# Attention inside a fused attention and two-layer MLP kernel: the product with v in fp32, 64 columns for each head, in place of three fp32r passes over 128 columns

## The chip, the cores and the metric

The kernel is written in Bass for one core of a Trainium2 chip. The core has TensorE (PE: matmuls and transposes), VectorE (DVE), ScalarE (ACT), GpSimd (POOL) and the queues of SyncE (SP), which issues the DMAs. The metric is the device time of one execution in microseconds (us). Two times are compared as medians over several runs.

## The reference

What is computed, for B = 4 batches, H = 8 heads, S = 576 positions, D = 64, all float32:

```python
scores = scale * np.matmul(q, k.transpose(0, 1, 3, 2))        # per batch and head, 576 x 576
x = (log1p(|i - j|) / log1p(max(i, 1)))[..., None]
bias = np.maximum(x @ w1 + b1, 0.0) @ w2                       # (576, 576, 8), the same for every batch
scores = scores + bias.transpose(2, 0, 1)[None]
attn = softmax(scores, axis=-1)                                # with 1e-9 added to the sum
x = np.matmul(attn, v)                                         # then (B*S, H*D) = (2304, 512)
h = np.maximum(np.maximum(x @ moe_w1, x @ moe_w2), x @ moe_w3) # 2304 x 768
y = h @ moe_w_out                                              # 2304 x 512
out = gelu_like(y @ moe2_w_in) @ moe2_w_out                    # inner width 2048, piecewise quadratic
```

## The kernel before, in words

The kernel has four stages that follow one another: the bias for all heads (to about 63 us), attention (to about 423 us), the first MLP and the second MLP. The change touches attention alone.

TensorE knows two ways of multiplying 32-bit numbers here. An fp32r operand is a number rounded to fewer bits; a product of two of them is one matmul. To keep precision, a number x is split into `hi` (x rounded) and `lo` (x minus hi, rounded), and a product is the sum of `hi*hi`, `hi*lo` and `lo*hi`. An fp32 operand goes in whole, and the trace shows two matmul records for one such product.

**Pairs and steps.** A (batch, head) is called a pair here, m = 0 to 31, and two neighbours (m even and odd) have the same batch and adjoining heads; i = m // 2 counts these. All engines run `step(m, par, i)` for m = -1 to 34, with par = m % 2. Steps -1 to 3 and 30 to 34 are written out, and steps 4 to 29 are a loop over i with two steps in its body (`steps`); in the loop semaphores are waited on against register values, and `carry` adds one `sem_inc` on several engines.

**One step on TensorE** is five tiles of query rows, t = 0 to 4 (the last has 64 rows). For each t, in order:

- scores of pair m: four matmuls of 288 columns (L1043), k_hi and k_lo against `q_s`, where `q_s` holds hi of q in partitions 0 to 63 and lo of q in 64 to 127. They all write the one place `score_ps()`, so each tile waits until DVE has read the tile before (`s_bias`);
- transposes of the normalised probabilities of pair m-1, four of 128x128 into one PSUM bank (L1055, slot `p0` to `p4`);
- at t = 0, 1, 2, transposes of q and k of pair m+1 (L975, L1071, slots `q`, `k`, `qk`), whose inputs `q_dup` and `k_dup` hold each row twice side by side;
- a share of the product with v (`output_share`, `outputs`, L988). `v_hi` and `v_lo` hold, for a block kt of keys, v of both heads with a zero block between them, so that a stationary 128x128 operand has v of one head in its own 64 columns and zeros in the other's. Nine such blocks (four for each head, and one in which the tails of both heads lie in 64 partitions each) times three passes times two column halves (256 and 320 columns, PSUM banks 6 and 7) make 54 matmuls for two pairs. They are dealt over t = 2, 3, 4 of the even step m = 2i and over t = 0 to 4 of the odd step that follows. After an even step come four transposes of the collected tails (`tail`, L1079).

The transposes use four PSUM banks, 2 to 5, by the tables `T_BANKS`; `before` finds the slot that held a bank last, and `open_slot` waits until DVE is done with it.

**The other engines.** DVE adds bias to the scores and finds the minimum (L818, two buffers `s_sb`, so it also waits for the exp two tiles ago). ACT takes the exp (L635). POOL normalises the probabilities (L512) and copies their last 64 columns to `p_tail` (L518). Each transposed slot is rounded by ACT to hi (`high`, L616) and then DVE subtracts to get lo (`low`, L802, for lo of q L804). POOL writes `q_dup` and `k_dup` (`dup`, L503) and splits v to `v_hi` (L530) and `v_lo` (L533). ACT copies finished outputs to `xT` (L653, L657). SP loads q and k two pairs ahead, v one double pair at a time into one buffer, and at each change of heads the bias (`load_bias`, L356).

Of the kernel before, what the change touches and what calls it, by code (L numbers as in the profile page):

```python
# [20 lines left out]
F32 = mybir.dt.float32  # L21
# [3 lines left out]
ds = bass.ds  # L25
# [5 lines left out]
def build(nc, q, k, v, w1, b1, w2, moe_w1, moe_w2, moe_w3, moe_w_out, moe2_w_in, moe2_w_out, out):  # L31
# [41 lines left out]
    with ctx:  # L73
# [9 lines left out]
        with att:  # L83
# [18 lines left out]
            v_hi = sb("v_hi", [P, 3 * T + 2, D], F32R, c=att)  # L102
            v_lo = sb("v_lo", [P, 3 * T + 2, D], F32R, c=att)
# [8 lines left out]
            p_hi = sb("p_hi", [P, 2, T, S], F32R, c=att)  # L112
            p_lo = sb("p_lo", [P, 2, T, S], F32R, c=att)
            pt_hi = sb("pt_hi", [P, S], F32R, c=att)
            pt_lo = sb("pt_lo", [P, S], F32R, c=att)
# [4 lines left out]
        with moe:  # L120
# [16 lines left out]
        O_AT = (3, 1)  # L137
# [21 lines left out]
        vv_in = sem("vv_in")  # L159
        dup_ok = sem("dup_ok")  # L160
        v_hi_ok = sem("v_hi_ok")
        v_ok = sem("v_ok")
        t_ps = sem("t_ps")
        t_hi = sem("t_hi")
        t_lo = sem("t_lo")
        tail_ps, tail_hi, tail_lo = sem("tail_ps"), sem("tail_hi"), sem("tail_lo")
# [35 lines left out]
        ORDER = ("p0", "q", "p1", "k", "p2", "qk", "p3", "p4")  # L202
        T_BANKS = (dict(zip(ORDER + ("tail",), (2, 3, 4, 5, 2, 3, 4, 5, 2))),
                   dict(zip(ORDER, (3, 4, 5, 2, 4, 5, 3, 4))))
        QK_ONLY = ("q", "k", "qk")
        P_ONLY = tuple(n for n in ORDER if n not in QK_ONLY)
        Q_AT, K_AT, QK_AT = 0, 1, 2

        def order_of(m):

            if not isinstance(m, int):
                return ORDER
            return QK_ONLY if m < 1 else P_ONLY if m >= PAIRS - 1 else ORDER

        def filled(m):

            if isinstance(m, int):
                return sum(len(order_of(n)) for n in range(-1, m))
            return len(ORDER) * m + (filled(4) - len(ORDER) * 4)

        def slot(m, name):

            return filled(m) + order_of(m).index(name)

        def before(m, par, i, name):


            bank = T_BANKS[par][name]
            names = order_of(m) + (("tail",) if par == 0 and later(m, 2) else ())
            earlier = names[:names.index(name)]  # L230
            while True:
                for n in reversed(earlier):
                    if T_BANKS[par][n] == bank:
                        return (tail_lo, i) if n == "tail" else (t_lo, slot(m, n) + 1)
                m, i, par = m - 1, i if par else i - 1, 1 - par
                if isinstance(m, int) and m < -1:
                    return None
                earlier = order_of(m) + (("tail",) if par == 0 and later(m, 2) else ())

        def steps(eng, body):  # L240

            def peeled(m):
                body(m, m % 2, m // 2)

            for m in range(-1, 4):
                peeled(m)
            with eng.Fori(2, PAIRS // 2 - 1) as i:
                body(2 * i, 0, i)
                body(2 * i + 1, 1, i)
            for m in range(PAIRS - 2, PAIRS + 3):  # L250
                peeled(m)

        def has(m, lag):

            return not isinstance(m, int) or 0 <= m - lag < PAIRS

        def later(m, first):

            return not isinstance(m, int) or m >= first
# [43 lines left out]
        passed = {name: sem(f"{name}_passed") for name in ("pe", "dve", "pool", "sp")}  # L303

        def carry(eng, m, name):


            if not isinstance(m, int):
                eng.sem_inc(passed[name], 1)

# [3 lines left out]
        def _(sp):  # L314
# [18 lines left out]
            def load_qk(b, hp, e, first=False):  # L333

                m = 2 * (B * hp + b) + e
                if not first:
                    sp.wait_ge(dup_ok, m - 1)
                    carry(sp, m, "sp")
                load(q, q_in, b, 2 * hp + e, e, qk_in[e], "(p t) d -> p t d")
                load(k, k_in, b, 2 * hp + e, e, qk_in[e], "(t p) d -> p t d")  # L340

            def load_v(b, hp):

                if not (isinstance(b, int) and b == 0 and hp == 0):
                    sp.wait_ge(v_ok, B * hp + b)
                    if not isinstance(b, int):
                        carry(sp, b, "sp")
                for h in range(2):
                    sp.dma_start(v_in[:, 2 * h:3 * T:3, :],
                                 v[b, 2 * hp + h, 0:MAIN, :].rearrange("(t p) d -> p t d", t=T)).then_inc(vv_in, 16)  # L350
                    sp.dma_start(v_in[h * HALF:(h + 1) * HALF, 3 * T + h, :],
                                 v[b, 2 * hp + h, MAIN:S, :]).then_inc(vv_in, 16)

            def load_bias(hp, e):
# [3 lines left out]
                sp.dma_start(bias_h[0:HALF, e, T, :], bias_d[MAIN:S, h, :]).then_inc(bias_in[e], 16)  # L358

            load_qk(0, 0, 0, True)  # L360
            load_qk(0, 0, 1, True)
            load_v(0, 0)


# [826 lines left out]
```

## Time and profile before

| | |
|---|---|
| median of 3 runs | 1139.0 us (1138.79 to 1141.09) |
| profiled execution, its own time | 1139.37 us |
| its span in the profile | 1137.6 us |
| granted TensorE clock, mean | 0.99 of full speed |
| steps 2 to 31 | one double step, even and odd, in 21.3 us |

The span is the time from the first to the last instruction on the core. A record of a matmul has a modelled end, which lies after the start of the next; so the time that a matmul takes in a stream is read from the distance between two starts, and from the share that says "busy" nothing can be read on how well TensorE is used.

### The profile page before, as it was taken

How to read it: one execution, taken by the hardware profiler on the slowest of the kernel's cores; microseconds unless marked ns; L12 is line 12 of the kernel's file. 1: busy time of each engine (PE TensorE's matmuls, PEld its weight loads, DVE VectorE, ACT ScalarE, POOL GpSimd, SP SyncE). 2: the span in 40 equal slices, each digit the busy share in tenths (PEclk: the TensorE clock that was granted, in tenths of full speed). 3: DMA queues.
4: the chain of work that ended last, by engine and by line, in shares of the span. 5: the costliest groups of instructions: out<-in, count | busy, mean ns of one | idle time of the engine just before them, and what ended most of it. 6: DMA issues, size and time to landing. Idle time of an engine off the chain costs nothing.

```text
span 1137.6 us, 21240 instructions
## 1 busy us (share of the span) xinstructions
PE 1091.7 (96%) x6872; PEld 998.1 (88%) x6872; DVE 632.1 (56%) x1441; ACT 575.0 (51%) x1210; POOL 341.9 (30%) x544
## 2 busy tenths in 40 slices
PE   6869999999999979999999999999999999999997
PEld 2358899899899879999999999999899989989996
DVE  8958888888888852323222222475444444444543
ACT  7957887887887853312121122464334343433432
POOL 5027767767767737400000003481000000000000
PEclk9979999999999999999999999999999999999999
DMA  4551141141141114200000002140101000010101
GB/s 136 210 186 42 48 130 42 47 130 42 47 130 42 28 32 131 93 1 1 0 0 0 0 0 75 56 130 1 29 1 28 0 17 11 0 28 0 29 1 28
DMA packets 80774, 55.30 MB, mean 49 GB/s; under 512 B 44896, under 2 KB 66400, under 8 KB 80736
## 3 DMA queue, kind: packets, MB, share of 16 engines
q1 hardware_dynamic: 80736, 54.82, 16.4%
q8 instruction: 21, 0.34, 0.1%
q14 instruction: 17, 0.14, 0.0%
HBM read 39.46 MB, written 15.34 MB: 48 GB/s over the span
## 4 chain that ended last, share of the span: by engine, by line
PE 86%; issue 2%; DVE 2%; POOL 1%; ACT 1%; ACTq 0%; DVEq 0%
PE ps L1095 37%; PE ps L1139 18%; PE ps L988 11%; PE ps L1043 7%; PE ps L1107 7%; PE ps L1055 5%; DVE s_sb L818 1%; PE ps L975 1%; PE ps L1071 1%; PE ps L1079 1%; ACT probs L635 0%; POOL w_lo L563 0%; DVE row_min L818 0%; POOL v_lo L533 0%; POOL probs L512 0%
## 5 line engine op out<-in xcount | busy, mean ns | idle before, releaser
L1095 PE MATMUL ps<-x_hi,w_hi 128*128 128x384 f32 x816 | 274.4, 336 | 3.8 <-DVE x_lo L860 3.5
L1095 PE MATMUL ps<-x_hi,w_lo 128*128 128x384 f32 x816 | 274.3, 336 | 0.0
L1095 PE MATMUL ps<-x_lo,w_hi 128*128 128x384 f32 x816 | 273.8, 336 | 0.0
L563 POOL TENSOR_TENSOR w_lo<-raw,w_hi 128x256 fp32r<-128x256 f32 x108 | 83.6, 804 | 274.4 <-ACT w_hi L671 274.2
L1095 PEld LDWEIGHTS ps<-x_hi,w_hi 128*128 128x128 f32 x816 | 153.8, 188 | 8.6 <-issue 3.7
L1095 PEld LDWEIGHTS ps<-x_lo,w_hi 128*128 128x128 f32 x816 | 153.6, 188 | 3.9
L1095 PEld LDWEIGHTS ps<-x_hi,w_lo 128*128 128x128 f32 x816 | 153.5, 188 | 0.0
L818 DVE CUSTOM_DVE_ANT_0 s_sb<-ps,bias_h 128x576 f32<-128x576 f32 (+1 forms) x160 | 120.3, 752 | 43.8 <-PE ps L1043 24.5
L512 POOL TENSOR_SCALAR probs<-probs,row_inv 128x512 f32<-128x512 f32 (+1 forms) x160 | 108.3, 692 | 91.6 <-DVE row_inv L792 91.6
L635 ACT ACTIVATE probs<-s_sb,row_min 128x576 f32<-128x576 f32 (+1 forms) x160 | 124.3, 777 | 19.2 <-DVE row_min L818 18.3
L616 ACT ACTIVATE p_hi<-ps 128x512 fp32r<-128x512 f32 (+1 forms) x160 | 88.7, 555 | 58.4 <-PE ps L1055 46.0
L1139 PE MATMUL ps<-w_hi,g_lo 128*128 128x512 f32 x288 | 113.9, 395 | 0.0
L1139 PE MATMUL ps<-w_lo,g_hi 128*128 128x512 f32 x288 | 113.6, 395 | 0.0
L1139 PE MATMUL ps<-w_hi,g_hi 128*128 128x512 f32 x288 | 112.6, 391 | 0.0
L802 DVE TENSOR_TENSOR p_lo<-ps,p_hi 128x512 fp32r<-128x512 f32 (+1 forms) x160 | 101.0, 632 | 8.1 <-ACT p_hi L616 5.6
L727 ACT ACTIVATE ta<-ps 128x384 f32<-128x384 f32 x96 | 47.0, 490 | 115.7 <-PE ps L1095 115.0
L907 DVE TENSOR_SCALAR tb<-ta 128x384 f32<-128x384 f32 x96 | 38.0, 396 | 113.9 <-ACT ta L727 112.1
L874 DVE TENSOR_TENSOR tb<-ps,ta 128x384 f32<-128x384 f32 x36 | 20.1, 557 | 144.5 <-PE ps L1095 144.5
L1055 PE MATMUL ps<-ident,probs 128*128 128x128 f32 (+1 forms) x640 | 92.5, 267 | 1.1 <-DVE p_lo L802 1.1
L1043 PE MATMUL ps<-k_hi,q_s 128*128 128x288 f32 (+1 forms) x320 | 75.8, 319 | 15.6 <-DVE row_min L818 13.3
L915 DVE TENSOR_TENSOR g_lo<-tb,g_hi 128x384 fp32r<-128x384 f32 x96 | 56.9, 593 | 58.5 <-ACT g_hi L737 58.5
L988 PE MATMUL ps<-p_hi,v_hi 128*128 128x256 f32 (+1 forms) x256 | 86.1, 336 | 1.4 <-POOL v_lo L533 1.4
(104 smaller groups left out, 2029.3 us busy)
## 6 DMA issues: line engine op xcount, KB each, us to landing
bias_scratch<-probs SPq DMA_DIRECT2D x36, 288.0 KB, 2.1
bias_h<-bias_scratch SPq DMA_DIRECT2D x7, 1152.0 KB, 5.9
raw<-in_moe_w_out SPq DMA_DIRECT2D x22, 256.0 KB, 3.0
raw<-in_moe_w SPq DMA_DIRECT2D x18, 256.0 KB, 3.0
out<-o_sb SPq DMA_DIRECT2D x36, 128.0 KB, 2.4
q_in<-in_q SPq DMA_DIRECT2D x32, 128.0 KB, 2.0
k_in<-in_k SPq DMA_DIRECT2D x32, 128.0 KB, 2.4
v_in<-in_v SPq DMA_DIRECT2D x32, 128.0 KB, 2.3
```

Source lines behind the costliest of these rows:

```text
L512: pool.tensor_scalar(pr, pr, row_inv[0:rows[t], par, t:t + 1], 1.0, ALU.mult, ALU.mult).then_inc(p_norm, 1)
L563: last = pool.tensor_tensor(w_lo[:, at + c:at + c + PIECE], raw[:, u % 2, c:c + PIECE], w_hi[:, at + c:at + c + PIECE].bitcast(F32), ALU.s ...
L616: last = act.activation(dst, src, ACT.Copy, scale=scale)
L635: act.activation(probs[0:n, par, t, :], s_sb[0:n, (par + t) % 2, :], ACT.Exp, scale=-1.0, bias=row_min[0:n, par, t:t + 1], accum_out=row_s ...
L802: last = dve.tensor_tensor(dst, src, hi.bitcast(F32), ALU.subtract)
L818: dve.tensor_tensor_reduce(halves(s_sb[0:n, (par + t) % 2, :]), score_ps()[0:n], halves(bias_h[0:n, par, t, :]), 1.0, 3.0e38, ALU.add, ALU ...
L988: last = pe.matmul(ps[:, bank, 0:cols.stop - cols.start], vx[:, at:at + 2, :].rearrange("p a d -> p (a d)"), tx[:, cols] if h is None else ...
L1043: last = pe.matmul(score_ps()[0:n, c, :], q_s[:, par, t * P:t * P + n], kx[:, par, c * HC:(c + 1) * HC], start=(part == 0), stop=(part == 1))
L1055: last = pe.transpose(ps[:, bank, c * n:(c + 1) * n], pr[:, c * P:(c + 1) * P], ident[0:n, 0:n])
L1095: last = pe.matmul(ps[:, bank, 0:BLK], w[:, at:at + P], x[:, kt, :], start=(kt == 0 and n == 0), stop=(kt == KT - 1 and n == 2))
L1107: last = pe.matmul(ps[:, Y_BANK + dt, 0:BLK], w[:, at:at + P], g[:, ft % 2, :], start=(opens and i == 0), stop=(closes and i == 2))
L1139: last = pe.matmul(ps[:, O_BANK + t, :], g[:, ft % 4, t * P:(t + 1) * P], w[:, wout_d(ft):wout_d(ft) + DM], start=(opens and i == 0), stop ...
```

## The change: what it does

- **The product with v** takes `v_in` as it is loaded and the transposed probabilities, both in fp32. Head 0 has a stationary operand of 128x64 that writes PSUM partitions 0 to 63, head 1 another that writes 64 to 127, in turn. Five blocks of keys (the last is the tail, with zeros in v for the other head's partitions) times two heads times two column halves make 20 products, 40 records, for two pairs. They are dealt by `SHARES`: t = 2 has block 0, t = 3 blocks 1 and 2, t = 4 blocks 3 and 4; the 256-column half in the odd step 2i+3, the 320-column half in the even step 2i+4, one step later than before.
- **p is copied, not split.** `p0` and `p2` are copied by ACT alone, `p1`, `p3`, `p4` and `tail` by DVE alone, to `p_t` and `pt_t`, which have two buffers. The v split on POOL is gone.
- **q is split ahead of its transpose.** POOL writes hi of q (320 elements a partition) to one half of `q_dup`, duplicates k as before, and subtracts to get lo of q in the other half. After the transpose ACT alone writes `q_s`; DVE's subtraction for q is gone. k is split as before.
- **Steps are written out**, all 36 of them, with constants in every wait. The four banks go round in the order of the slots; a slot waits for the copy of the slot four before it, on a count of ACT's or DVE's (`t_act`, `t_dve`).
- **SP** loads v into two buffers and waits for the outputs of the double pair before the last (`o_ps`); this wait stands ahead of the loads of q and k and of the bias in its queue.

The core of the diff:

```diff
-            v_in = sb("v_in", [P, 3 * T + 2, D], c=att)
+            v_in = sb("v_in", [P, 2, 2, NT, D], c=att)
-            p_hi = sb("p_hi", [P, 2, T, S], F32R, c=att)
-            p_lo = sb("p_lo", [P, 2, T, S], F32R, c=att)
+            p_t = sb("p_t", [P, 2, 2, T, S], c=att)
+            pt_t = sb("pt_t", [P, 2, S], c=att)
+        SHARES = {2: (0,), 3: (1, 2), 4: (3, 4)}
...
+        BY_ACT = ("p0", "p2", "q", "k", "qk")
+        BY_DVE = ("p1", "p3", "p4", "tail", "k", "qk")
+        SLOTS = [(m, name) for m in STEPS for name in names_of(m)]
+        T_BANKS = 4
+        def t_bank(m, name):
+            return 2 + SLOT[m, name] % T_BANKS
...
+            def load_v(i):
+                if i >= 2:
+                    sp.wait_ge(o_ps, 2 * (i - 2) + 2)
...
+            for i in range(PAIRS // 2):
+                if i:
+                    load_v(i)
+                for e in range(2):
+                    if i + 2 < PAIRS // 2:
+                        load_qk(2 * (i + 2) + e)
+                    if i % B == B - 1 and i + 1 < PAIRS // 2:
+                        sp.wait_ge(s_bias, NT * (2 * i + e + 1))
+                        load_bias((i + 1) // B, e)
...
+                pool.tensor_scalar(q_dup[:, par, :, 0, :].bitcast(F32R), q_in[:, par, :, :], 1.0, 1.0,
+                                   ALU.mult, ALU.mult).then_inc(q_hi_ok, 1)
+                pool.tensor_scalar(k_dup[:, par, :, :, :],
+                                   k_in[:, par, :, :].unsqueeze(2).broadcast_to([P, NT, 2, D]), 1.0, 1.0,
+                                   ALU.mult, ALU.mult)
+                pool.wait_ge(q_hi_ok, m + 1)
+                pool.tensor_tensor(q_dup[:, par, :, 1, :], q_in[:, par, :, :], q_dup[:, par, :, 0, :],
+                                   ALU.subtract).then_inc(dup_ok, 1)
...
-                    pool.tensor_scalar(v_hi[:, :, :], v_in[:, :, :], 1.0, 1.0, ALU.mult, ALU.mult).then_inc(v_hi_ok, 1)
-                    pool.tensor_tensor(v_lo[:, :, :], v_in[:, :, :], v_hi[:, :, :].bitcast(F32),
-                                       ALU.subtract).then_inc(v_ok, 1)
...
-                        if t == Q_AT + 1:
-                            qs = q_s[HALF:P, e, 0:MAIN]
-                            low("q", [(qs, ps[HALF:P, T_BANKS[par]["q"], 0:MAIN], -SCALE, qs)])
...
+                    if has(m, 1) and f"p{t}" in BY_DVE:
+                        src = ps[:, t_bank(m, f"p{t}"), :]
+                        i = (m - 1) // 2
+                        last = copy(f"p{t}", p_t[:, i % 2, e, :, t * P:t * P + n],
+                                    src[:, 0:T * n].rearrange("p (c n) -> p c n", c=T))
...
+                def outputs(i, half, kts):
+                    bank, cols = O_BANKS[half]
+                    for kt in kts:
+                        if kt == 0:
+                            if half == 0:
+                                pe.wait_ge(vv_in[i % 2], 64 * (i // 2 + 1))
+                                pe.wait_ge(t_act, ACT_COUNT[2 * i + 2, "p2"])
+                                pe.wait_ge(t_dve, DVE_COUNT[2 * i + 2, "tail"])
+                            if i >= 1:
+                                pe.wait_ge(o_ok, 2 * (i - 1) + half + 1)
+                        for h in range(2):
+                            last = pe.matmul(ps[h * HALF:(h + 1) * HALF, bank, 0:cols.stop - cols.start],
+                                             v_in[:, i % 2, h, kt, :],
+                                             pt_t[:, i % 2, cols] if kt == T else p_t[:, i % 2, h, kt, cols],
+                                             start=(kt == 0), stop=(kt == T))
+                    if kts[-1] == T:
+                        last.then_inc(o_ps, 1)
...
+                    if par == 1 and has(m, 3):
+                        outputs((m - 3) // 2, 0, SHARES[t])
+                    if par == 0 and has(m, 4):
+                        outputs((m - 4) // 2, 1, SHARES[t])
...
+            for m in STEPS:
+                step(m)
```

## Rows read from the trace of the kernel before

**Rows 1.** The page: busy engines, and the granted clock in 40 slices.
```profile
PE 1091.7 (96%) x6872; PEld 998.1 (88%) x6872; DVE 632.1 (56%) x1441; ACT 575.0 (51%) x1210; POOL 341.9 (30%) x544
PEclk9979999999999999999999999999999999999999
```

**Rows 2.** Windows: stretch, busy us of each engine (instructions), granted clock, DMA.
```profile
200.00:300.00 100.00, 98.22 (x752) 91.21 (x752) 87.01 (x225) 81.10 (x199) 72.00 (x123) 1.00 0.25 69
88.00:92.00 4.00, 2.90 (x21) 2.35 (x22) 3.22 (x11) 2.73 (x7) 3.69 (x7) 1.00 0.01 4
```

**Rows 3.** Timeline of PE, scores at four tiles: start, us, operation, count.
```profile
200.09 0.53 PE L1043 MATMUL ps<-k_hi,q_s 128*128 128x288 f32 x2 [0.20 <-DVE row_min L818]
...
217.68 0.49 PE L1043 MATMUL ps<-k_hi,q_s 128*128 128x288 f32 x2
...
219.53 0.54 PE L1043 MATMUL ps<-k_hi,q_s 128*128 128x288 f32 x2 [0.22 <-DVE row_min L818]
...
221.40 0.53 PE L1043 MATMUL ps<-k_hi,q_s 128*128 128x288 f32 x2 [0.20 <-DVE row_min L818]
```

**Rows 4.** Timeline of DVE: the tile of scores of 219.53 as DVE takes it.
```profile
220.59 0.75 DVE L818 CUSTOM_DVE_ANT_0 s_sb<-ps,bias_h 128x576 f32<-128x576 f32 x1
```

**Rows 5.** Timeline of PE, tiles 1, 2 and 3 of an odd step.
```profile
209.87 0.60 PE L1055 MATMUL ps<-ident,probs 128*128 128x128 f32 x4
210.30 0.60 PE L975 MATMUL ps<-ident,k_dup 128*128 128x128 f32 x4
...
211.62 0.42 PE L1043 MATMUL ps<-k_hi,q_s 128*128 128x288 f32 x2
...
212.15 0.60 PE L1055 MATMUL ps<-ident,probs 128*128 128x128 f32 x4
212.68 0.27 PE L1071 MATMUL ps<-ident,q_dup 64*128 64x64 f32 x1
212.79 0.22 PE L1071 MATMUL ps<-ident,k_dup 64*128 64x64 f32 x1
212.95 0.39 PE L988 MATMUL ps<-pt_hi,v_hi 128*128 128x256 f32 x1
213.17 0.28 PE L988 MATMUL ps<-pt_lo,v_hi 128*128 128x256 f32 x1
213.29 0.29 PE L988 MATMUL ps<-pt_hi,v_lo 128*128 128x256 f32 x1
...
214.38 0.60 PE L1055 MATMUL ps<-ident,probs 128*128 128x128 f32 x4
...
215.11 0.31 PE L988 MATMUL ps<-p_hi,v_lo 128*128 128x320 f32 x1
215.25 0.31 PE L988 MATMUL ps<-p_hi,v_hi 128*128 128x320 f32 x1
```

**Rows 6.** Timeline of PE, one tile of the bias stage, into four column groups.
```profile
58.03 1.30 PE L948 MATMUL ps<-xT,w2b 128*32 128x288 f32 x16 [0.29 <-ACT xT L583]
```

**Rows 7.** Groups by line, 200 to 300 us, of DVE and POOL.
```profile
L802 DVE TENSOR_TENSOR p_lo<-ps,p_hi 128x512 fp32r<-128x512 f32 x38 | 26.1, 686 | 0.3
L804 DVE SCALAR_TENSOR_TENSOR q_s<-ps,q_s 64x512 fp32r<-64x512 f32 x10 | 7.0, 695 | 0.3
L533 POOL TENSOR_TENSOR v_lo<-v_in,v_hi 128x896 fp32r<-128x896 f32 x5 | 10.6, 2110 | 0.9 <-POOL v_hi L530 0.9
L503 POOL TENSOR_SCALAR q_dup<-q_in 128x640 f32<-128x640 f32 x10 | 7.2, 720 | 0.0
```

**Rows 8.** Timeline of PE at the end of attention.
```profile
412.37 0.51 PE L988 MATMUL ps<-p_hi,v_hi 128*128 128x256 f32 x1 [1.35 <-POOL v_lo L533]
...
422.67 0.31 PE L988 MATMUL ps<-pt_hi,v_lo 128*128 128x320 f32 x1
426.48 0.66 PE L1095 MATMUL ps<-x_hi,w_hi 128*128 128x384 f32 x1 [3.50 <-DVE x_lo L860]
```

**Rows 9.** Timeline of the SP queue at a change of heads.
```profile
227.77 0.57 SPq L356 DMA_DIRECT2D bias_h<-bias_scratch  x1
```

More of the change, by code:

```diff
@@ L215, in filled @@
[L215 to L251, printed above, removed]
-        def has(m, lag):
-            return not isinstance(m, int) or 0 <= m - lag < PAIRS
-        def later(m, first):
-            return not isinstance(m, int) or m >= first
+        STEPS = range(-1, PAIRS + 3)
@@ new lines, in build, with names_of @@
+        Q_AT, K_AT, QK_AT = 0, 1, 2
+        BY_ACT = ("p0", "p2", "q", "k", "qk")
+        BY_DVE = ("p1", "p3", "p4", "tail", "k", "qk")
+        def has(m, lag):
+            return 0 <= m - lag < PAIRS
+        def names_of(m):
+            for t in range(NT):
+                if has(m, 1):
+                    yield f"p{t}"
+                if has(m, -1) and t in (Q_AT, K_AT, QK_AT):
+                    yield {Q_AT: "q", K_AT: "k", QK_AT: "qk"}[t]
+            if m % 2 == 0 and has(m, 2):
+                yield "tail"
@@ L607, in _, with step, turned, output @@
                 bias_copy(s, s % 4, NSUP // 4 - 1)
-            def step(m, par, i):
+            def step(m):
+                par = m % 2
                 e = 1 - par
-                def high(name, outs):
-                    act.wait_ge(t_ps, slot(m, name) + 1)
-                    for dst, src, scale in outs:
-                        last = act.activation(dst, src, ACT.Copy, scale=scale)
-                    last.then_inc(t_hi, 1)
+                def turned(name):
+                    act.wait_ge(t_ps, SLOT[m, name] + 1)
+                    return ps[:, t_bank(m, name), :]
+                def output(i, half):
+                    bank, cols = O_BANKS[half]
+                    act.wait_ge(o_ps, 2 * i + half + 1)
+                    act.activation(xT_flat[:, i * S + cols.start:i * S + cols.stop],
+                                   ps[:, bank, 0:cols.stop - cols.start], ACT.Copy).then_inc(o_ok, 1)
@@ L663, in _ @@
-            steps(act, step)
+                            src = turned("qk")
+                            act.activation(q_s[:, e, MAIN:S], src[:, 0:HALF], ACT.Copy, scale=-SCALE)
+                            act.activation(k_hi[:, e, MAIN:S], src[:, HALF:2 * HALF], ACT.Copy).then_inc(t_act, 1)
+                    if t == O_AT:
+                        if par == 0 and has(m, 4):
+                            output(m // 2 - 2, 0)
+                        if par == 1 and has(m, 5):
+                            output((m - 1) // 2 - 2, 1)
@@ L664, in _ @@
+            for m in STEPS:
+                step(m)
+            output_last = PAIRS // 2 - 1
+            bank, cols = O_BANKS[1]
+            act.wait_ge(o_ps, PAIRS)
+            act.activation(xT_flat[:, output_last * S + cols.start:output_last * S + cols.stop],
+                           ps[:, bank, 0:cols.stop - cols.start], ACT.Copy).then_inc(o_ok, 1)
             act.wait_ge(o_ok, PAIRS)
@@ L854, in _ @@
-            steps(dve, step)
+                            last = dve.tensor_copy(pt_t[:, i % 2, MAIN:S], src[:, T * n:NT * n])
+                        last.then_inc(t_dve, 1)
+            for m in STEPS:
+                step(m)
             dve.wait_ge(o_ok, PAIRS)
@@ L1080, in step @@
                                             p_tail[:, t, :, :].rearrange("p a d -> p (a d)"), ident[:, :])
-                    last.then_inc(tail_ps, 1)
-            steps(pe, step)
+                    last.then_inc(t_ps, 1)
+            for m in STEPS:
+                step(m)
             pe.wait_ge(o_ok, PAIRS)
```

278 lines of the change are left out of this document (83 added, 195 removed).

## The prediction

> **What bounds the kernel now.** I read the page first. TensorE is busy for 96% of the span and no other engine for more than 56% [rows 1]. In the attention stage, which is all that the change touches, the windows show a PE that is 98% busy, with DVE at 87%, ACT at 81% and POOL at 72%, at full clock [rows 2]. So the stage hangs on TensorE, but three engines are close behind. Whether a busy PE is working or waiting is read from the starts in its timeline. Scores at the same tile of two even steps start at 200.09 and 221.40 us: a double step takes 21.31 us [rows 3]. The stage has 15 of them in steady state (steps 2 to 31), 320 us of the 1137.6.
>
> Two kinds of tile make up a double step. At tiles 0 and 1 of an even step PE has no product with v to do, and it waits for DVE: the starts are 1.85 and 1.87 us apart, with an idle time put down to row_min each time [rows 3]. This is a loop: scores (0.53 us of PE when nothing hinders them, 211.62 to 212.15 [rows 5]), then DVE starts on them, then PE may write the next. DVE took the scores of 219.53 at 220.59 and PE went on at 221.40 [rows 3, 4], so from DVE's start to PE's next start 0.81 us pass. At the other eight tiles the products with v fill the time and PE goes from one thing to the next.
>
> **The change part by part.**
>
> *The products removed.* Starts of neighbouring passes are 0.12 us apart for 256 columns (213.17 to 213.29) and 0.14 to 0.15, I take 0.145, for 320 columns (215.11 to 215.25) [rows 5]. 27 of each for a double step: 3.24 + 3.92 = 7.2 us.
>
> *The products added.* In fp32 a record streams at half the rate: four transposes of 128 columns take 209.87 to 210.30, 0.43 us, so 0.107 us for 128 columns of one record [rows 5]. A product is two records, so 256 columns take 0.43 us and 320 take 0.53. Alone, 20 products would be 10 x (0.43 + 0.53) = 9.6 us, more than what goes. Side by side on their own columns the two heads would be half, 4.8 us. The nearest row for that is the bias stage: eight fp32 products of 288 columns, 16 records into four groups of 32 columns, stand in 1.30 us [rows 6]. At the rate just found one record of 288 is 0.24 us and 16 in a row 3.84 us. So column groups do run beside one another, with different moving data, in the same bank. That was four groups of 32; two of 64 is the same thing at another width, and I take 4.8 us.
>
> *What a change of tiling costs.* This is the unknown. The trace shows a change of row tiling: transposes of 128 rows from 212.15 end their stream at 212.58, and those of 64 rows start at 212.68, 0.10 later. They end at about 212.85; the third pass of the product behind them starts at 213.29, 0.44 later, where two passes are 0.24: 0.20 to get back to 128x128. Where no tiling changes, transposes from 214.38 end at 214.81 and the third pass starts at 215.11, 0.30 for two of 0.145, so nothing [rows 5]. So I price a share of the product with v, entered and left, at 0.10 + 0.20 = 0.30 us. There are six shares in a double step (tiles 2, 3 and 4, twice). At tiles 2 and 4 a change out of 64 rows is there already and merges with the new one. The bounds: 0 if 64-column tiles need no change, and 0.55 if, besides, the second head trails the first by a record (0.21 to 0.27) at the end of each share.
>
> The Trainium skill, "TensorEngine Tiling (Array Packing)", Key Properties, speaks against the change here: another tile of the same mode is free, but a new mode drains TensorE. It has no figure for that; the 0.10 and 0.20 above agree with it, for rows. By its table of theoretical speedup (up to 2x for a dimension of 64) alone, the products would take 4.8 us and the changes nothing.
>
> *The new double step.* The rows give transposes 0.43, the pair of small transposes with the step into 64 rows 0.27 (212.58 to 212.85), scores 0.53, or 0.63 after a wait for DVE, when the weights are not in ahead (an estimate: 1.87 between the two waiting starts of rows 3 is 0.63 of scores, 0.43 to the start on DVE, and 0.81). The last tile, with its 64-row transposes, is 0.95 without products, by my reading of the same timeline, and 0.43 more for the tails in the even step.
> - Tiles 0 and 1 in both steps are now in the loop with DVE. Before, the tile at 219.53 lost about 0.1 because DVE was still at the last lo. That work is gone, so 1.80 in place of 1.86: 4 x 1.80 = 7.20.
> - Even step, 320 columns: tile 2 has 0.63 + 0.43 + 0.27 + 0.53 + 0.30 = 2.16; tile 3 has 0.96 + 1.07 + 0.30 = 2.33; tile 4 has 0.95 + 0.43 + 1.07 + 0.30 = 2.75. Together 7.24.
> - Odd step, 256 columns: 2.06, 2.11 and 2.10, together 6.27.
>
> In all 20.7 us. In the same way of counting the old step comes out 0.1 low (a wait here and there), so I take 20.85, which is 0.46 less than 21.31. Times 15: -6.9 us. The 2.4 us that the streams save per double step are given back as 1.8 of tiling changes, and as tiles 0 and 1 of the odd step, whose products used to cover the loop with DVE and now don't.
>
> *DVE* loses two of five p_lo (0.69 each) and the lo of q (0.70 and a small one) each step [rows 7]; the rest become copies, for which I take the subtraction's time. From 87% of 10.66 us, 9.3, it goes to about 7.1 in a step of 10.4. *ACT* loses p1, p3, p4 and the tail and has less to do as well. *POOL* loses v_lo (2.11 every second step) and v_hi [rows 7]. For q it gains a rounding of 320 elements and a subtraction of 320, which by v_lo's rate is 0.75, and loses the 0.72 of q_dup: about +0.5 a step against -1.5. All of this is behind TensorE and costs or gives nothing, beyond the 0.06 in the loop. What waits on POOL (p_norm for tile 0 of the next step) had over a microsecond to spare.
>
> *The written-out steps* drop register arithmetic and one sem_inc an engine. The steps written out already are not visibly quicker except for about 0.1 at tile 0; I take 0. A bigger program means more fetching of instructions; nothing in the trace bounds that, 0 again.
>
> *SP.* The wait on o_ps now stands before eight DMA issues, some 0.55 us each by the row of another (0.57), and at a change of heads before the bias. Bias went out at 227.77 for a step that began at 239.0 and its data took some 6 us [rows 9]. It will go out about 4.5 us later, with a step that is shorter by 0.2: some 1 us is left. Three such places; cost 0, at worst 3 x 1 us.
>
> *The ends.* At the start the second tile waits for the bias, whatever else; 0 to -0.7, I take -0.3. At the end PE waited for v_lo before 412.37, ran the passes until 422.67 plus 0.15, partly at half clock, and the MLP began at 426.48 [rows 8]. Now nothing waits for v, and after the last transposes there are 4.8 us of products, of which the first half waits for the copy of the tails (about 1.3 us). I take -2.5, between 0 and -4.
>
> Sum, against the profiled execution's 1139.4: -6.9 - 0.3 - 2.5 = -9.7, so 1129.7. It stands 0.4 above the median; that makes 1129.
>
> **The rivals.**
> 1. *Changing the tiling costs nothing.* Then a double step has tiles of 1.80 (the loop holds all but two), 2.03 and 2.5: about 19.0 us. 15 x -2.3 - 3 gives 1102. For it: the scores of the last tile, labelled 128*64, come behind 128*128 products with no gap. Against: those are fp32r at position 0, and may not be tiled at all; and the row tiles do pay. Cases in between, at 0.15 a share, give 1115.
> 2. *The second head trails and the drain is dearer*, 0.6 us a share. Six times 0.3 more than I took: 22.6 us, 15 x 1.3 - 3 gives 1156. It decides from about 0.40 a share, where the time is as before. For it: the bias tile's last record starts 0.89 after its first (1.30 less 0.41 for the record itself), where four rounds of 0.24 would have 0.72 [rows 6]; so the groups do not start together.
> 3. *The two heads do not overlap at all* (the other side, and far). 4.8 us more per double step: 25.6, 15 x 4.3 - 2 gives about 1200. Against it stands rows 6 alone. The Trainium skill, "TensorE: Matmul & The Clock Gate", What overlaps and what doesn't, says that weight loads overlap matmuls only when the row group differs; here both heads have the same rows. Taken at its word, with loads of 64 columns exposed, this would be rival 2 or 3; rows 6 has one row group as well, and overlaps.
> 4. *The clock.* PE has more gaps, and the granted clock could fall to 1.2 GHz, as in the drain. At 88 to 92 us PE is busy for 2.9 us of 4 and the clock stays at 1.00 [rows 2]. If it fell for good, well over 1200.
>
> **How the numbers follow.** Forecast, 0.2 to 0.45 us a share: 0.50. Rival 1: 0.24. Rival 2: 0.14. Rival 3: 0.10. Rival 4: 0.02. The forecast's own range is 1121 to 1139. For the range over all, rival 3 and 4 and the far end of rival 1 stay outside: 1103 to 1152. Within 0.2% (2.3 us), about what a measurement of this kernel can tell from no change, are the top of the forecast's band and the bottom of rival 2: 0.12. Faster: rival 1 and most of the band, 0.68. Slower: 0.20.
>
> **What would show it.** In the profile after: two records of 256 columns for each head with starts that make 0.43 us a block, not 0.85; gaps of 0.1 before and 0.2 after each share; scores at tiles 0 and 1 of both steps 1.8 us apart with an idle time before them that ends on row_min; even steps longer than odd ones, by about 1 us; no wait of DVE for bias. The prediction is wrong if a share costs much more or less than 0.3, or if PE waits for a bank, for p_norm or for v.

## The result, and the profile after

The changed kernel takes 1124.1 us (median of 4 runs, 1122.6 to 1125.5) against 1139.3 us of the kernel before beside it: a ratio of 0.9864, 95% interval 0.9851 to 0.9876. It is 15.2 us faster, where 10 were forecast; 1124.1 lies inside the whole range and inside the forecast's own 1121 to 1139.

The page of the changed kernel, whose profiled execution took 1122.62 us with a span of 1120.8:

```profile
PE 1076.4 (96%) x6648; PEld 918.9 (82%) x6648; DVE 559.7 (50%) x1313; ACT 515.2 (46%) x1082; POOL 312.7 (28%) x544
PEclk9979999999999999999999999999999999999999
```

By its share PE is as busy as in [rows 1], and the clock is the same. Only windows over the attention stage tell the two apart (stretch, busy us of PE, PEld, DVE, ACT, POOL, granted clock, DMA share and GB/s):

```profile
200.00:300.00 100.00, 98.35 (x710) 70.93 (x708) 68.22 (x196) 66.07 (x168) 66.10 (x128) 1.00 0.27 72
```

Beside [rows 2], DVE went from 87 to 68, ACT from 81 to 66, POOL from 72 to 66. PE is "98% busy" in both and says nothing; its weight loads fell from 91 to 71. What the stage takes is read from the starts. PE in the changed kernel, an odd step from 200.40, then an even one from 210.05 (start, us, operation, count):

```profile
200.40 0.51 PE L955 MATMUL ps<-k_hi,q_s 128*128 128x288 f32 x2
...
202.13 0.53 PE L955 MATMUL ps<-k_hi,q_s 128*128 128x288 f32 x2
...
203.78 0.53 PE L955 MATMUL ps<-k_hi,q_s 128*128 128x288 f32 x2
...
205.79 0.53 PE L955 MATMUL ps<-k_hi,q_s 128*128 128x288 f32 x2
...
206.43 0.60 PE L967 MATMUL ps<-ident,probs 128*128 128x128 f32 x4
206.96 1.08 PE L927 MATMUL ps<-p_t,v_in 128*64 128x256 f32 x8
207.97 0.48 PE L955 MATMUL ps<-k_hi,q_s 128*64 128x288 f32 x2
...
208.65 0.46 PE L967 MATMUL ps<-ident,probs 64*128 64x64 f32 x4
...
210.05 0.53 PE L955 MATMUL ps<-k_hi,q_s 128*128 128x288 f32 x2
...
211.80 0.53 PE L955 MATMUL ps<-k_hi,q_s 128*128 128x288 f32 x2
...
213.45 0.53 PE L955 MATMUL ps<-k_hi,q_s 128*128 128x288 f32 x2
...
215.57 0.54 PE L955 MATMUL ps<-k_hi,q_s 128*128 128x288 f32 x2
...
217.97 0.48 PE L955 MATMUL ps<-k_hi,q_s 128*64 128x288 f32 x2
...
220.73 0.51 PE L955 MATMUL ps<-k_hi,q_s 128*128 128x288 f32 x2
```

The double step takes 20.33 us (200.40 to 220.73), 0.98 less than the 21.31 of [rows 3]. Its ten tiles, against the prediction's terms:

| tile | odd: forecast, measured | even: forecast, measured |
|---|---|---|
| 0 | 1.80, 1.73 | 1.80, 1.75 |
| 1 | 1.80, 1.65 | 1.80, 1.65 |
| 2 | 2.06, 2.01 | 2.16, 2.12 |
| 3 | 2.11, 2.18 | 2.33, 2.40 |
| 4 | 2.10, 2.08 | 2.75, 2.76 |

A share of the product can be read at 206.96. The transposes before it end their stream at 206.43 + 0.43 = 206.86, so the way in costs 0.10. Two blocks of 256 columns are 0.85 us, scores 0.53 and the step into 64 rows 0.09; from 206.96 to 208.65 are 1.69, which leaves 0.22 for the way out. At tile 2 (205.21, not shown) the same sum leaves 0.27. A share costs 0.32 to 0.37, where I took 0.30. What the time of the way out is spent on is not shown: about 0.10 of it lies between the first two pairs of scores behind a share, and scores that have waited for DVE, with no change of tiling before them, show the same 0.10.

Where the 16.8 us between the two spans (1137.6 and 1120.8) come from, by starts of PE in both traces:

| stretch | before | after | difference |
|---|---|---|---|
| first scores to the start of step 3 | 34.0 | 31.2 | -2.8 |
| steps 3 to 30, 14 double steps | 298.2 | 286.8 | -11.4 |
| step 31 to the first matmul of the MLP | 27.8 | 25.2 | -2.5 |
| the rest | 777.6 | 777.6 | 0.0 |

The first row is in part chance. Its steps 0 and 1 take 22.8 us here, but 24.1 in the profile of bias_first and 21.9 in that of tail_moved (both below), whose code for these steps is nearly the same; in this stretch the granted clock changes between its two levels at different places (at 75 to 79 us it is 0.87 before and 0.50 after, at 82 to 85 us 0.53 and 0.91).

Fourteen times 0.98 would be 13.7. The missing 2.2 us are a new wait. The chain that ended last, in order of time, at the first change of heads in the changed kernel:

```profile
143.28 0.60 SPq L311
143.88 0.04 issue
143.92 6.03 DMA bias_h<-bias_scratch
149.96 0.02 issue
149.98 0.76 DVE s_sb L752
```

The queue of SP ahead of it, from its timeline:

```profile
137.97 0.37 SPq L304 DMA_DIRECT2D v_in<-in_v  x1
...
142.72 0.52 SPq L288 DMA_DIRECT2D k_in<-in_k  x1
143.28 0.60 SPq L311 DMA_DIRECT2D bias_h<-bias_scratch  x1
```

The bias goes out 5.3 us after v, behind eight issues (four of v, four of q and k), and its data land 6 us later; DVE waits 2.26 us for them at 149.98. That step and the ones at the two other changes of heads are 1.13, 0.84 and 0.19 us longer than their like.

### The profile page after: what moved, and what is told of

Same layout as the page of the kernel before. It is cut to its first block, busy times and chain, and to the rows that moved or that the text cites. A ratio compares the mean times of both kernels' runs of the same rounds, so it can differ in the third digit from the quotient of the medians.

```text
span 1120.8 us, 18895 instructions
## 1 busy us (share of the span) xinstructions
PE 1076.4 (96%) x6648; PEld 918.9 (82%) x6648; DVE 559.7 (50%) x1313; ACT 515.2 (46%) x1082; POOL 312.7 (28%) x544
## 3 DMA queue, kind: packets, MB, share of 16 engines
q1 hardware_dynamic: 80736, 54.82, 16.8%
## 4 chain that ended last, share of the span: by engine, by line
PE 82%; issue 3%; DVE 3%; DMA 2%; SPq 1%; ACT 0%; POOL 0%; ACTq 0%; DVEq 0%
PE ps L1008 38%; PE ps L1052 18%; PE ps L955 7%; PE ps L1020 7%; PE ps L927 6%; PE ps L967 4%; DVE s_sb L752 2%; DMA bias_h<-bias_scratch 2%; PE ps L911 1%; DVE p_t L741 1%; PE ps L983 1%; POOL w_lo L500 0%; SPq L286 0%; SPq L306 0%; ACT w_hi L611 0%
## 5 line engine op out<-in xcount | busy, mean ns | idle before, releaser
L955 PE MATMUL ps<-k_hi,q_s 128*128 128x288 f32 (+1 forms) x320 | 84.7, 347 | 14.3 <-DVE row_min L752 10.8
L955 PEld LDWEIGHTS ps<-k_hi,q_s 128*128 128x128 f32 (+1 forms) x320 | 45.3, 181 | 61.8 <-DVE row_min L752 39.9
L927 PE MATMUL ps<-p_t,v_in 128*64 128x320 f32 (+1 forms) x512 | 82.4, 424 | 1.0 <-DVE pt_t L761 1.0
L677 ACT ACTIVATE g_hi<-tb 128x384 fp32r<-128x384 f32 x96 | 50.4, 525 | 64.2 <-DVE tb L845 64.2
```

The source lines that it names most:

```text
L677: act.activation(g_hi[:, ft % 4, :], tb[:, :], ACT.Copy).then_inc(d_g_hi, 1)
L927: last = pe.matmul(ps[h * HALF:(h + 1) * HALF, bank, 0:cols.stop - cols.start], v_in[:, i % 2, h, kt, :], pt_t[:, i % 2, cols] if kt == T ...
L955: last = pe.matmul(score_ps()[0:n, c, :], q_s[:, par, t * P:t * P + n], kx[:, par, c * HC:(c + 1) * HC], start=(part == 0), stop=(part == 1))
```

## The experiments

Eleven runs. Each ratio is to the kernel before, run beside it on the same chip.

### The two heads on the same columns

```diff
-                            last = pe.matmul(ps[h * HALF:(h + 1) * HALF, bank, 0:cols.stop - cols.start],
+                            last = pe.matmul(ps[0:HALF, bank, 0:cols.stop - cols.start],
...
-                                             start=(kt == 0), stop=(kt == T))
+                                             start=(kt == 0 and h == 0), stop=(kt == T and h == 1))
```

(A memset of the PSUM columns that nobody writes any more stands at the start of DVE. This kernel does not compute the same thing: it leaves the two heads unparted, and what it writes is their sum.)

> The changed kernel, with the products of both heads written to PSUM partitions 0 to 63, so that both use the same 64 columns of TensorE (the output is then the sum of two heads and half of it is missing; every instruction is still there). Theory A, the two heads run beside one another on their own columns: that ends, a block of keys costs 0.85 and 1.07 us in place of 0.43 and 0.53, a double step goes from 20.3 to about 25.1 us, and the time from 1124 to about 1197. Rival B, the gain came from the work taken off DVE, ACT and POOL, and the products cost the same however they are placed: 1124, within 3 us.

1197.6 us, ratio 1.0492 (1.0471 to 1.0512). Theory A, to within a microsecond. Tile 3 of an odd step, PE:

```profile
205.39 0.60 PE L968 MATMUL ps<-ident,probs 128*128 128x128 f32 x4
205.91 1.94 PE L928 MATMUL ps<-p_t,v_in 128*64 128x256 f32 x8
207.78 0.48 PE L956 MATMUL ps<-k_hi,q_s 128*64 128x288 f32 x2
```

The eight records stand 1.87 us before the next scores, where with two column groups they stand 1.01 (206.96 to 207.97). The difference, 0.86, is two blocks at 0.43. Every matmul is still there with the same operands; only the place of head 1's output was changed (and with it the flags that open and close the sum). So it is shown that the heads run beside one another and that the change hangs on it: without it the kernel would be 4.9% slower than before. Whether it is the shared columns or the shared place in PSUM that puts the products in a row was not parted.

### The heads in turn within a share

```diff
-                    for kt in kts:
...
-                        for h in range(2):
+                    for h in range(2):
+                        for kt in kts:
                             last = pe.matmul(
```

> The changed kernel, but within a share all blocks of head 0 come before those of head 1; same work, same placement. If TensorE takes its matmuls strictly in order and can only overlap neighbours, the shares with two blocks (four of six) lose most of the overlap: up to 0.43 or 0.53 us more for each, 1.9 us for a double step, about 1150. If column groups have queues of their own that hold a few records, nothing changes: 1124.

1123.6 us, ratio 0.9859 (0.9834 to 0.9884): no difference. The steps are 9.66 and 10.69, as in the changed kernel. PE at the start of the share of tile 3, in a window that ends at 206.20:

```profile
206.16 0.44 PE L928 MATMUL ps<-p_t,v_in 128*64 128x256 f32 x2
```

Two records stand in these 0.44 us, where one alone is 0.43: they start together, within 0.02 us. In the program four records of head 0 come first. All eight take 1.09 us, as before (1.08), where on one column group they took 1.94; so the two that start together are of different heads, and the overlap does not need neighbours in the program, at least up to four records.

### The kernel before, with its steps written out

```diff
-            for m in range(-1, 4):
-                peeled(m)
-            with eng.Fori(2, PAIRS // 2 - 1) as i:
-                body(2 * i, 0, i)
-                body(2 * i + 1, 1, i)
-            for m in range(PAIRS - 2, PAIRS + 3):
+            for m in range(-1, PAIRS + 3):
                 peeled(m)
```

> The kernel before with steps 4 to 29 written out as well (on TensorE, DVE, ACT and POOL), nothing else. My forecast put this part at nothing: 1139, within 2. If the register arithmetic and the waits on registers are a part of the gain, tiles 0 and 1 of the even steps come down from 1.85 to about 1.75 and the time to 1136. If fetching the longer program costs, slower than 1141.

1135.2 us, ratio 0.9947 (0.9929 to 0.9966), 5.6 us less (4 to 8 by the interval; the spans of the two profiles differ by 4.2). My zero was wrong. The double step is 21.00, and all of the 0.3 is in tiles 0 and 1 of the even step: 1.65 and 1.75 in place of 1.85 and 1.87. PE, then DVE, then GpSimd in this kernel, at those tiles:

```profile
195.31 0.43 PE L1038 MATMUL ps<-k_lo,q_s 128*128 128x288 f32 x2
...
197.06 0.43 PE L1038 MATMUL ps<-k_lo,q_s 128*128 128x288 f32 x2
```
```profile
195.87 0.76 DVE L813 CUSTOM_DVE_ANT_0 s_sb<-ps,bias_h 128x576 f32<-128x576 f32 x1 [0.78 <-issue]
...
196.56 0.37 DVE L784 TENSOR_SCALAR row_den<-row_sum 128x2 f32<-128x2 f32 x1
...
197.04 0.67 DVE L797 TENSOR_TENSOR p_lo<-ps,p_hi 128x512 fp32r<-128x512 f32 x1
197.63 0.75 DVE L813 CUSTOM_DVE_ANT_0 s_sb<-ps,bias_h 128x576 f32<-128x576 f32 x1
```
```profile
195.97 0.94 POOL L525 TENSOR_SCALAR v_hi<-v_in 128x896 fp32r<-128x896 f32 x1
```

And DVE and GpSimd at the same two tiles of the kernel before, ahead of the row at 220.59 [rows 4]:

```profile
218.71 0.76 DVE L818 CUSTOM_DVE_ANT_0 s_sb<-ps,bias_h 128x576 f32<-128x576 f32 x1 [0.80 <-ACT probs L635]
...
219.40 0.45 DVE L789 TENSOR_SCALAR row_den<-row_sum 128x2 f32<-128x2 f32 x1
219.87 0.17 DVE L792 RECIPROCAL row_inv<-row_den 128x2 f32<-128x2 f32 x1
219.98 0.69 DVE L802 TENSOR_TENSOR p_lo<-ps,p_hi 128x512 fp32r<-128x512 f32 x1
```
```profile
218.88 0.93 POOL L530 TENSOR_SCALAR v_hi<-v_in 128x896 fp32r<-128x896 f32 x1
```

At tile 0 DVE waits for the scores. It begins 0.13 us after their end here (195.87 less 195.74) and 0.27 in the kernel before (218.71 less 218.44); besides, the second pair of scores follows the first by 0.27 here and by 0.33 there.

At tile 1 DVE waits for nothing. Between the scores of tile 0 and those of tile 1 it stands idle for 0.04 us in all, in either kernel. What sets this tile is DVE's own chain: scores of tile 0, the sums of the rows (`row_den`, `row_inv`), the lo of p, scores of tile 1. Of this chain one piece differs, `row_den`, with 0.45 and 0.37 us; the same instruction takes 0.16 otherwise. In the two traces it takes over 0.22 us 32 times. Each time it ends 0.02 to 0.03 us behind an instruction of GpSimd, and 29 times that is `v_hi` (here at 219.81 and 196.91). So DVE's chain is held until GpSimd is through with `v_hi`. The next scores of TensorE follow DVE's start by 0.82 in both kernels.

### Written out, with the loop's sem_incs

```diff
         def carry(eng, m, name):
-            if not isinstance(m, int):
+            if not isinstance(m, int) or 4 <= m < PAIRS - 2:
                 eng.sem_inc(passed[name], 1)
```

> The kernel before with all steps written out, but with the sem_incs that the loop had (one after most waits on TensorE, DVE, GpSimd) kept in steps 4 to 29. Written out without them it took 1135.2. If the sem_incs made DVE late for the scores (0.22 to 0.28 us after their last column in the loop, 0.04 to 0.13 when written out), the time goes back to about 1140 and tiles 0 and 1 to 1.85 us. If the waits against register values did, it stays at 1135 and the tiles at 1.65 and 1.75.

1139.0 us, ratio 1.0003 (0.9994 to 1.0013): all of the gain is gone. Tiles 0 and 1 take 1.75 and 1.89, and the double step 21.27. So it is the sem_incs. The one on DVE stands between its wait for the scores and the instruction, and what it costs there is read where DVE has nothing else to do. At tile 3 of an odd step the scores end at 191.92 in this kernel and DVE begins at 192.14, 0.22 later; written out without the sem_incs it is 191.90 and 191.94, 0.04 later. (The kernel before has 0.22 too. TensorE's products hide it at that tile.)

At tile 1 DVE's chain is again without a gap: `row_den` is held until `v_hi` ends on GpSimd, which now is 0.13 us later against DVE's start on tile 0. DVE and GpSimd:

```profile
175.44 0.51 DVE L784 TENSOR_SCALAR row_den<-row_sum 128x2 f32<-128x2 f32 x1
...
176.65 0.75 DVE L813 CUSTOM_DVE_ANT_0 s_sb<-ps,bias_h 128x576 f32<-128x576 f32 x1
```
```profile
174.99 0.94 POOL L525 TENSOR_SCALAR v_hi<-v_in 128x896 fp32r<-128x896 f32 x1
```

Once in this trace `v_hi` came early enough to hold up nothing. There DVE waits for the scores, which end at 346.88, and begins 0.23 us behind them; its two starts are 1.83 us apart all the same. (The row names an exp of ACT, but the exp that this tile waits for ended at 344.75.)

```profile
345.28 0.76 DVE L813 CUSTOM_DVE_ANT_0 s_sb<-ps,bias_h 128x576 f32<-128x576 f32 x1 [1.10 <-issue]
...
345.96 0.16 DVE L784 TENSOR_SCALAR row_den<-row_sum 128x2 f32<-128x2 f32 x1
...
347.11 0.76 DVE L813 CUSTOM_DVE_ANT_0 s_sb<-ps,bias_h 128x576 f32<-128x576 f32 x1 [0.19 <-ACT probs L630]
```

So two limits lie close together at tile 1. The loop of scores takes 1.83 with the sem_incs and 1.65 without (as tile 0 of before_unrolled and tile 1 of the changed kernel show); DVE's chain with `v_hi` takes 1.88 and 1.76. The sem_incs lengthen both. Those on the four engines were not parted. In the loop tile 0 took 1.85, 0.1 more than here, and an odd step 0.04 less; so the waits against registers may move something from tile to tile, but over the kernel they show no cost.

### Written out, and q split ahead on GpSimd

The edit is `dup` as in the change, with DVE's lo of q left out and a bare `sem_inc` on t_lo in its place.

> The kernel before, steps written out, and q split on GpSimd ahead of its transpose as in the change, with the product with v still in three fp32r passes. The written-out kernel took 1135.2, with tile 1 of the even step at 1.75 us, held by DVE's lo of q and of p. Theory A: without the lo of q that tile takes 1.65, 0.1 less for a double step, 1133.7; GpSimd's longer work is hidden. Rival: GpSimd is late for p_norm or the transposes of q wait for it, slower than 1136.

1135.2 us, ratio 0.9952 (0.9934 to 0.9971), the same as without it. Tile 1 stays at 1.75. Theory A was wrong about that tile and the rival wrong about GpSimd: this part of the change is worth nothing, in either direction. The trace says why theory A fell. DVE's lo of q stands behind its scores of tile 1, so what it delays is DVE's start on tile 2: that comes 0.03 us after the end of the scores in place of 0.51, and tile 2 takes 2.60 in both kernels, filled by TensorE's products. The chain ahead of tile 1 was not touched (`row_den` is still held, 0.38).

### More work for DVE at tile 1

```diff
+                        if t == 1:
+                            copy("p1", spare[:, 0:T * n], src[:, 0:T * n])
                         last = copy(f"p{t}", p_t[
```

> The changed kernel with one more copy of 512 elements on DVE at tile 1 of each step (0.6 us, into a spare tile nobody reads), which gives DVE about the work there that the lo of q gave it. Theory A, DVE is close enough to the loop of the scores that its relief counts: DVE comes 0.3 us late to tile 2, of which PE's longer tile hides a part, about +0.1 a step, 1127. Rival, all of DVE's relief is hidden behind TensorE: 1124.

1124.9 us, ratio 0.9865 (0.9842 to 0.9888). No tile changes (1.73, 1.65, 2.01, 2.18, 2.08 in the odd step), so theory A falls; the profile is longer than the changed kernel's in its first steps and in its waits for the bias only. This work too stands behind the scores of tile 1: DVE comes 0.23 us later to tile 2, and TensorE's longer tile hides it. What stands ahead of tile 1 in DVE's chain was not tested by a run.

### Two and four shares a step

```diff
-        SHARES = {2: (0,), 3: (1, 2), 4: (3, 4)}
+        SHARES = {3: (0, 1, 2), 4: (3, 4)}            # two_shares
+        SHARES = {1: (0,), 2: (1,), 3: (2,), 4: (3, 4)}   # four_shares
```

> The changed kernel with the product with v in two shares a step (three blocks at tile 3, two at tile 4) in place of three. Theory A, each share costs 0.33 us of changed tiling, and a tile can't be shorter than the 1.65 us of the loop with DVE: tile 2 goes from 2.01 and 2.12 to 1.65, tile 3 from 2.18 and 2.40 to 2.61 and 2.93, in all +0.13 for a double step, 1126. Rival, no such floor: the two changes of tiling saved make it 0.6 a double step faster, 1115.

> The changed kernel with the product with v in four shares a step (a block each at tiles 1, 2 and 3, two at tile 4). Theory A, a share costs 0.33 us: tile 1 goes from 1.65 to 2.17 and 2.27, tile 3 from 2.18 and 2.40 to 1.75 and 1.87, in all +0.2 for a double step, 1127. Rival, a change of tiling is free and the work would only fill the wait for DVE at tile 1: tile 1 takes 1.82 and 1.93, -0.5 a double step, 1117.

Two shares: 1127.2 us, ratio 0.9896 (0.9870 to 0.9923), with steps of 9.72 and 10.76. Four shares: 1126.9 us, ratio 0.9891 (0.9868 to 0.9914), with steps of 9.74 and 10.77. The rivals' 1115 and 1117 are out both times. That either is slower than three shares is read from the steps (0.15 and 0.18 more for a double step), as the intervals of the ratios overlap with the changed kernel's. In two_shares tile 2 of the odd step takes 1.66 and tile 3 takes 2.61. PE in four_shares, tile 1 of an odd step:

```profile
204.03 0.53 PE L955 MATMUL ps<-k_hi,q_s 128*128 128x288 f32 x2
...
205.10 0.60 PE L911 MATMUL ps<-ident,k_dup 128*128 128x128 f32 x4
205.63 0.65 PE L927 MATMUL ps<-p_t,v_in 128*64 128x256 f32 x4
206.21 0.53 PE L955 MATMUL ps<-k_hi,q_s 128*128 128x288 f32 x2
```

The transposes end their stream at 205.53, the products begin 0.10 later, and the next scores 0.58 after that, of which the block is 0.43. A tile that had 0.26 us to spare (0.16 of waiting, and the 0.10 between its pairs of scores) grew by 0.53 with one block of 0.43, so the share costs 0.36. One share less saves nothing either, since tile 2 then stands against the loop with DVE.

### The bias first in SP's queue

```diff
-                if i:
-                    load_v(i)
                 for e in range(2):
-                    if i + 2 < PAIRS // 2:
-                        load_qk(2 * (i + 2) + e)
                     if i % B == B - 1 and i + 1 < PAIRS // 2:
                         sp.wait_ge(s_bias, NT * (2 * i + e + 1))
                         load_bias((i + 1) // B, e)
+                    if i + 2 < PAIRS // 2:
+                        load_qk(2 * (i + 2) + e)
+                    if e == 0 and i:
+                        load_v(i)
```

> The changed kernel with another order in SP's queue: at each step the bias first, then q and k, and the load of v after those of the even pair. In the changed kernel three odd-to-even steps at changes of heads are 1.13, 0.84 and 0.19 us longer than the others, with DVE waiting for the bias. If that is the place of v's wait in the queue, these go: 1122. If the bias is late for another reason (its own 6 us of transfer), no change: 1124.

1121.7 us, ratio 0.9831 (0.9813 to 0.9848), and the three steps are 10.68 like the rest. The bias goes out at 138.66 where it went out at 143.28:

```profile
138.66 0.58 SPq L311 DMA_DIRECT2D bias_h<-bias_scratch  x1
```

### The tails' transposes in a tile that waits

```diff
+                    if t == 0 and par == 1 and has(m, 3):
+                        bank = open_slot("tail")
+                        for c in range(T):
+                            last = pe.transpose(ps[:, bank, c * P:(c + 1) * P],
+                                                p_tail[:, c, :, :].rearrange("p a d -> p (a d)"), ident[:, :])
+                        last.then_inc(t_ps, 1)
                     output_share(t)
-                if par == 0 and has(m, 2):
-                    bank = open_slot("tail")
...
```

with the slot, its copy on DVE (now at tile 1) and the waits on it moved along, on top of the order of SP's queue above.

> The order of SP's queue as in bias_first (1121.7), and the four transposes of the tails moved from the end of the even step into tile 0 of the odd step, where TensorE waits for DVE; their copy moves to tile 1. Theory A, the tiles at 1.75 and 1.65 are the loop of scores and hold 0.26 us of waiting each: the last tile of the even step loses 0.43, tile 0 of the odd step gains 0.1 to 0.15, so 0.3 less for a double step, 1117. Rival, the starts there are set by TensorE's own work: what is taken from one tile is added to the other, 1121.7.

> The same kernel as bias_first, beside tail_moved on the same chip, so that the two can be compared: 1121.7, within 1.

1116.2 us, ratio 0.9804 (0.9791 to 0.9817), against 1121.7 us, ratio 0.9848 (0.9835 to 0.9862), on the same chip. PE around it:

```profile
216.79 0.53 PE L955 MATMUL ps<-k_hi,q_s 128*128 128x288 f32 x2
...
217.85 0.60 PE L911 MATMUL ps<-ident,q_dup 128*128 128x128 f32 x4
218.28 0.60 PE L990 MATMUL ps<-ident,p_tail 128*128 128x128 f32 x4
218.64 0.52 PE L955 MATMUL ps<-k_hi,q_s 128*128 128x288 f32 x2
```

Tile 0 of the odd step goes from 1.73 to 1.85 with 0.43 us more in it, and tile 4 of the even step from 2.76 to 2.35. Over 14 double steps that is 4.3 us less between steps 3 and 31; the two profiles differ by 2.2 more in the steps before, where profiles of like kernels scatter as much. This kernel beats both of the others, the changed one by 8 us.

## Why the prediction was right, and where it was off

**The streams, 7.2 us for 4.8.** Right. The four groups of 32 columns in [rows 6] were a fair measure for two of 64; one_group shows what the other end of the bound costs. Its time was forecast as about 1200 (rival 3) and measured as 1197.6.

**The change of tiling, 0.30 us a share.** Right that it costs, and nearly right in size (0.32 to 0.37). The row-tile changes of [rows 5] were the right rows to price it by. Rival 1 (free) and rival 2 (0.6) are out. The rule that a new tiling mode drains TensorE (the Trainium skill, "TensorEngine Tiling (Array Packing)", Key Properties) agrees with four_shares, where one share more costs 0.36 us; no run shows whether a drain is what that time goes to. The second head does not trail the first by a record: pairs of records start within 0.02 us of each other.

**Tiles 0 and 1, "1.80 in place of 1.86".** Here the step was mis-sized. They measure 6.78 together against 7.20, 0.42 a double step, and this with my allowance of 0.15 is why 20.85 became 20.33. The reason given was right for tile 1, and its price too small. DVE was indeed still at its last lo when the scores of 219.53 were ready: it has no gap from 218.71 to 220.59. But the tile stood 0.22 above the 1.65 of the bare loop, and not 0.06 to 0.1. What I missed is that `row_den` in this chain was held by `v_hi` on GpSimd, and that the chain ended late on the loop's sem_incs besides. With `v_hi` and the lo of p0 gone, DVE stands idle for 0.64 us between the scores of tiles 0 and 1, and the loop of scores alone sets 1.65. Which of the two takes tile 1 from 1.75 to 1.65 no run parts: by the rows `row_den` at its usual 0.16 would shorten the chain to about 1.55 and be enough by itself (an estimate). At tile 0 the reason does not hold: there DVE waited, and its late start and the late second pair of scores went with the sem_incs.

**"The written-out steps ... I take 0".** This is the step that failed. On the kernel before they are 5.6 us by the medians and 4.2 by the profiles, by way of tiles 0 and 1, and it is the sem_incs, not the register arithmetic. I had even looked at the steps written out already and found "about 0.1 at tile 0", and did not multiply: in the changed kernel four tiles of a double step stand in that loop. What the sem_incs would cost there was not measured.

**The ends.** The end was forecast at -2.5 and is -2.5: PE's last product ends at 406.2, where it was 423.0, and nothing waits for v. The start was taken at -0.3 and is -2.8. I missed that step 2 no longer has any product (it goes from 10.41 to 8.45), as the product comes one step later; the step this adds at the end hid in time that was waiting before. The other 0.8 lies in steps 0 and 1, which have no product in either kernel and scatter by more than that from profile to profile.

**SP's queue, "cost 0, at worst 3 x 1 us".** It cost 2.2, in the place and by the mechanism named. Delay and transfer were read right: the bias goes out 4.6 us later than when it is first in the queue (143.28 and 138.66), where I took 4.5, and its data take 6. The slack was read wrong. The stretch that the bias has is an odd step, and that went from 10.71 to 9.65, 1.06 shorter and not 0.2; my own terms for its tiles already said so.

**DVE, ACT and POOL** went down as forecast (DVE to 68% where 7.1 of 10.4 was said) and are behind TensorE everywhere but in the loop of scores.

In sum, of the 16.8 us between the spans 13.7 are the double steps, 2.8 the start and 2.5 the end, less 2.2 of waiting for the bias. Of the 13.7 the written-out steps make 4.3 if they are worth the same 0.31 a double step as in the kernel before. The remaining 9.4 hang on the two heads side by side, with the tiling changes taking back about 2 us a double step. The split between their parts (products, single copies in place of hi and lo, no `v_hi`) was not measured, since one needs the other. That the time fell inside the forecast's band is luck in part: my sum had the double steps some 7 us too dear and the start 2.5, and the bias 2.2 too cheap.

## What to carry to other kernels

Two products with 64 output columns each, in fp32 and on their own column groups, can replace three fp32r passes over a padded 128: count the columns streamed, then add a third of a microsecond for every stretch in another tiling, and keep these stretches few and long as far as the other limits of a tile allow (two longer shares gained nothing here). When a loop of two engines sets the pace of a tile, look at what stands between the wait and the instruction it is for (a sem_inc there is paid each time around), and then at whether the second engine waits at all: at tile 1 it was busy throughout, and one small instruction in its chain was held by a third engine. And put work with free timing into the tiles that wait: 0.43 us of transposes cost 0.12 there.

## What the runs showed of the hardware that was not expected

- A `sem_inc` of its own between DVE's wait and the instruction behind it, with others like it on PE and GpSimd: where DVE has nothing else to do (tile 3 of an odd step) it starts 0.22 us after the matmul's end in place of 0.04, and the kernel takes 1139.0 us in place of 1135.2.
- A small DVE instruction of 0.16 us (`row_den`, two elements a partition) takes 0.37 in before_unrolled, 0.45 in the kernel before and 0.51 in before_unrolled_carry while GpSimd runs `v_hi`, and ends 0.02 to 0.03 us behind it each time.
- Matmuls for one column group can run beside matmuls for the other that stand four records later in the program: two records start within 0.02 us in heads_in_turn, and the share takes 1.09 us, as against 1.08 with the heads in turn for each block.
- The way from 128x128 into tiles of 64 columns costs 0.10 us, and the way back to fp32r scores 0.22 to 0.27 us, of which 0.10 is also seen at scores that have waited.
